# Quotient by remainder kept in PSUM, three banks for the first up-projection, v transposed mid-step, tokens stationary in the last product

## The chip, the cores and the metric

The kernel runs on one core of a Trainium2 chip. The metric is the device time of a run in microseconds. The engines are PE (TensorE, with PEld its weight loads), DVE (VectorE), ACT (ScalarE), POOL (GpSimd) and SP, which only issues transfers here.

## The reference

Channel attention over 6016 tokens of 256 channels, then two feed-forward layers of width 2048:

```python
qn = q / (norm(q, axis=tokens) + 1e-6);  kn = k / (norm(k, axis=tokens) + 1e-6)
x = v @ softmax(kn.T @ qn / tau)              # softmax with + 1e-9 in its divisor
h = x @ w_in1
P = a0 + a1*h + a2*h**2 + a3*h**3
Q = 1.0 + abs(b0)*abs(h) + abs(b1)*h**2
y = (P / (Q + 1e-6)) @ w_out1
h = y @ w_in2
out = (h * clip(h + 3, 0, 6) / 6) @ w_out2
```

All is float32. The attention matrix is folded into the first weight, so that v goes straight into the first up-projection.

## The kernel before

Products that must be exact to float32 are made of three matmuls: each operand is split into a rounded high part and the rest as a low part (`_hi`, `_lo`), and hi*hi, hi*lo and lo*hi are summed in PSUM (`split_product`, lines 334 to 336).

The first 66 us compute q'k, the softmax and the first columns of the folded weight. Then come steps t = 0, 1, ... over 13 blocks of tokens: one of 256, ten of 512, one of 384, one of 256. A step has 16 slots j, one for each chunk of 128 of the 2048 hidden features. The hidden features lie on the partitions, the tokens along the free axis. Each engine runs its own list, written out by hand, and counting semaphores tie the lists; a loop on the engine repeats the steps 3 to 9, the others are unrolled.

First stage, block t, chunk j: PE makes h in one of the two banks of H1 (`up1`, six matmuls). ACT reads it three times: T = a3*h + a2 (L563), SQ = |b1|*h*h (L565), AB = |b0|*|h| (L567). DVE makes T*h (`horner_2`, L750), (T + a1)*h (`horner_1`, L756) and SQ + AB (`q_body`, L764; on POOL, L295, in step 1). ACT takes the reciprocal square root of Q and squares it, which gives an approximate 1/Q in Y (L574, L580). DVE makes S = (T + a0)*Y (L771), E = Q*Y (L777) and G = (2 - E)*S (L784), one Newton step. ACT rounds G to g1_hi (L586), DVE subtracts to g1_lo (L792; on POOL, L301, for blocks 0 and 1). PE adds g1 times a part of w_out1 into YP (`down1`, six matmuls). T, SQ and g1 have four buffers, Y, AB and G two. These run with lags of 1, 2, 3 and 5 slots behind chunk j (`LAG_ROOT`, `LAG_NEWTON`, `LAG_SPLIT1`, `LAG_DOWN1`).

When all 16 chunks of a block are in YP, it is split to yT_hi (ACT, L605) and yT_lo (DVE, L804). Second stage, six slots behind (`SHIFT2`): `up2` into one of two banks of H2, R = relu(h + 3) (ACT, L592), R = min(R, 6)*h (DVE `gate2`, L798), g2_hi (ACT, L598), g2_lo (POOL, L307), and `down2`, which adds weights times tokens into OP, features on the partitions, three slots later. At the end of a block ACT scales OP into oT (L614), PE transposes it back into OP (`transpose_out`, L458), ACT copies it to o_tok (L621) and SP stores it.

v of the next block is transposed by PE at the end of a step into H1 (`transpose_v`, L370) and split by ACT (L540) and DVE (L724); there the first stage of the next block starts afresh. PSUM has eight banks, two for each of H1, H2, YP and OP.

## Time and profile before

| | |
|---|---|
| median of 3 runs | 1241.63 us (1241.12 to 1242.3) |
| span of the profiled execution | 1240.4 us |
| PE busy | 1165.5 us, 94%, 5440 matmuls |
| PEld busy | 954.5 us, 77% |
| DVE busy | 1156.9 us, 93%, 1723 instructions |
| ACT busy | 961.1 us, 77%, 1782 instructions |
| POOL busy | 360.6 us, 29%, 276 instructions |
| chain that ended last | PE 41%, DVE 37%, issue 18%, ACT 3% |

Busy time is an average over all stages. A matmul's row lasts until its result is out, so rows of matmuls overlap: their rate is read from start to start. Rows of DVE and ACT overlap their successor too, by 0.07 to 0.1 us, where it does not wait for them. In the timeline a row can stand for several instructions (x2).

### The profile page before, as it was taken

The page shows a single profiled execution, that of the slowest core. Times are in us where ns is not written, and L with a number is a line of the kernel's source. Part 1 is how long each engine was busy: PE and PEld are TensorE (multiplying, and loading weights), DVE is VectorE, ACT ScalarE, POOL GpSimd, SP SyncE. Part 2 cuts the span into 40 slices and gives each one's busy share as a digit, 9 for nine tenths or more (in the row PEclk, how much of TensorE's full clock was granted, in tenths as well). Part 3 has the DMA queues.
Part 4 walks back from the last instruction along what each step waited for, and adds up shares of the span by engine and source line. Part 5 has one row for each costly group of instructions (what it writes and reads, how often), then busy time and mean ns, then how long its engine had stood idle before and what let it go on. Part 6 is the DMA issues. An engine that isn't in the chain of part 4 may idle for free.

```text
span 1240.4 us, 17387 instructions
## 1 busy us (share of the span) xinstructions
PE 1165.5 (94%) x5440; PEld 954.5 (77%) x5440; DVE 1156.9 (93%) x1723; ACT 961.1 (77%) x1782; POOL 360.6 (29%) x276
## 2 busy tenths in 40 slices
PE   7876788899999999999999999999999999999998
PEld 6755566787787787787787787787787787888898
DVE  5779999999999999999999999999999999999872
ACT  6566787888887887887887887887887887787864
POOL 2146576222222222222222222222222222222334
PEclk9887899999999999999999999999999999999999
DMA  9730000000000000000000000000000000000000
GB/s 319 265 111 1 18 1 1 1 26 1 1 34 1 0 34 0 0 34 0 0 34 0 0 34 0 0 34 0 0 34 1 1 31 1 1 26 1 18 1 22
DMA packets 16210, 33.65 MB, mean 27 GB/s; under 512 B 1824, under 2 KB 6176, under 8 KB 15904
## 3 DMA queue, kind: packets, MB, share of 16 engines
q1 hardware_dynamic: 16160, 33.04, 7.5%
q8 instruction: 24, 0.39, 0.1%
q14 instruction: 26, 0.21, 0.1%
HBM read 26.87 MB, written 6.16 MB: 27 GB/s over the span
## 4 chain that ended last, share of the span: by engine, by line
PE 41%; DVE 37%; issue 18%; ACT 3%; DMA 0%; DVEq 0%; SPq 0%; POOL 0%; ACTq 0%
DVE T L771 7%; PE H L334 6%; DVE G L784 6%; DVE T L750 6%; PE H L336 6%; PE H L335 6%; DVE SQ L764 5%; DVE R L798 5%; DVE g_lo L792 4%; PE OP L343 3%; PE OP L334 3%; PE OP L336 3%; PE OP L335 3%; PE YP L334 3%; PE YP L336 3%
## 5 line engine op out<-in xcount | busy, mean ns | idle before, releaser
L307 POOL TENSOR_TENSOR g_lo<-R,g_hi 128x512 fp32r<-128x512 f32 (+2 forms) x208 | 267.1, 1285 | 754.9 <-ACT g_hi L598 754.9
L563 ACT ACTIVATE T<-H,coef 128x512 f32<-128x512 f32 (+2 forms) x208 | 153.0, 735 | 161.0 <-PE H L336 160.9
L777 DVE SCALAR_TENSOR_TENSOR Y<-SQ,Y 128x512 f32<-128x512 f32 (+2 forms) x208 | 206.0, 991 | 0.5
L334 PE MATMUL H<-vT_hi,wf_hi 128*128 128x512 f32 (+2 forms) x416 | 159.8, 384 | 20.6 <-DVE T L756 15.2
L334 PE MATMUL H<-yT_hi,wu_hi 128*128 128x512 f32 (+2 forms) x416 | 157.7, 379 | 11.2 <-DVE R L798 10.5
L764 DVE TENSOR_TENSOR SQ<-SQ,AB 128x512 f32<-128x512 f32 (+2 forms) x192 | 167.4, 872 | 0.0
L334 PE MATMUL YP<-g_hi,wd_hi 128*128 128x512 f32 (+2 forms) x416 | 160.0, 385 | 6.3 <-DVE yT_lo L804 5.6
L771 DVE SCALAR_TENSOR_TENSOR T<-T,coef,Y 128x512 f32<-128x512 f32 (+2 forms) x208 | 163.0, 784 | 0.0
L334 PE MATMUL OP<-g_hi,wd_hi 128*128 128x512 f32 (+2 forms) x416 | 156.8, 377 | 1.8 <-ACT o_tok L621 1.5
L336 PE MATMUL YP<-g_hi,wd_lo 128*128 128x512 f32 (+2 forms) x416 | 157.0, 377 | 0.0
L335 PE MATMUL YP<-g_lo,wd_hi 128*128 128x512 f32 (+2 forms) x416 | 156.9, 377 | 0.0
L335 PE MATMUL H<-vT_lo,wf_hi 128*128 128x512 f32 (+2 forms) x416 | 156.3, 376 | 0.0
L336 PE MATMUL H<-vT_hi,wf_lo 128*128 128x512 f32 (+2 forms) x416 | 156.0, 375 | 0.0
L336 PE MATMUL H<-yT_hi,wu_lo 128*128 128x512 f32 (+2 forms) x416 | 155.4, 373 | 0.0
L336 PE MATMUL OP<-g_hi,wd_lo 128*128 128x512 f32 (+2 forms) x416 | 155.4, 373 | 0.0
L335 PE MATMUL H<-yT_lo,wu_hi 128*128 128x512 f32 (+2 forms) x416 | 155.3, 373 | 0.0
L335 PE MATMUL OP<-g_lo,wd_hi 128*128 128x512 f32 (+2 forms) x416 | 155.2, 373 | 0.0
L798 DVE SCALAR_TENSOR_TENSOR R<-R,H 128x512 f32<-128x512 f32 (+2 forms) x208 | 130.0, 625 | 21.9 <-ACT R L592 21.7
L750 DVE TENSOR_TENSOR T<-T,H 128x512 f32<-128x512 f32 (+2 forms) x208 | 130.0, 625 | 18.6 <-ACT AB L567 18.5
L756 DVE SCALAR_TENSOR_TENSOR T<-T,coef,H 128x512 f32<-128x512 f32 (+2 forms) x208 | 142.5, 685 | 0.5
L784 DVE SCALAR_TENSOR_TENSOR G<-Y,T 128x512 f32<-128x512 f32 (+2 forms) x208 | 142.9, 687 | 0.0
L574 ACT ACTIVATE Y<-SQ 128x512 f32<-128x512 f32 (+2 forms) x208 | 125.4, 603 | 19.1 <-DVE G L784 18.5
(89 smaller groups left out, 2259.6 us busy)
## 6 DMA issues: line engine op xcount, KB each, us to landing
qk<-in_q SPq DMA_DIRECT2D x23, 256.0 KB, 5.6
qk<-in_k SPq DMA_DIRECT2D x23, 256.0 KB, 7.0
v_raw<-in_v SPq DMA_DIRECT2D x10, 512.0 KB, 3.6
out<-o_tok SPq DMA_DIRECT2D x10, 512.0 KB, 3.7
w_raw_b<-in_moe_w_out SPq DMA_DIRECT2D x8, 512.0 KB, 5.7
w_raw_a<-in_moe_w_in SPq DMA_DIRECT2D x1, 2048.0 KB, 11.5
w_raw_b<-in_moe_w_in SPq DMA_DIRECT2D x4, 512.0 KB, 6.1
v_raw<-in_v SPq DMA_DIRECT2D x2, 256.0 KB, 7.1
```

The costliest lines, as they stand in the source:

```text
L307: nc.gpsimd.tensor_tensor(g2_lo[:, j % 4, 0:w], R[:, j % 4, 0:w], g2_hi[:, j % 4, 0:w].bitcast(fp32), ALU.subtract).then_inc(g2_lo_done, 1)
L334: nc.tensor.matmul(psum, w_hi, x_hi, start=first, stop=False)
L335: nc.tensor.matmul(psum, w_hi, x_lo, start=False, stop=False)
L336: return nc.tensor.matmul(psum, w_lo, x_hi, start=False, stop=last)
L563: nc.scalar.activation(T[:, j % 4, 0:w], H1[:, j % 2, 0:w], ACT.Identity, bias=A2, scale=A3)
L750: nc.vector.tensor_tensor(T[:, j % 4, 0:w], T[:, j % 4, 0:w], H1[:, j % 2, 0:w], ALU.mult)\
L756: nc.vector.scalar_tensor_tensor(T[:, j % 4, 0:w], T[:, j % 4, 0:w], A1, H1[:, j % 2, 0:w], ALU.add, ALU.mult).then_inc(t3_done, 1)
L764: nc.vector.tensor_tensor(SQ[:, j % 4, 0:w], SQ[:, j % 4, 0:w], AB[:, j % 2, 0:w], ALU.add)\
L771: nc.vector.scalar_tensor_tensor(T[:, j % 4, 0:w], T[:, j % 4, 0:w], A0, Y[:, j % 2, 0:w], ALU.add, ALU.mult).then_inc(s_done, 1)
L777: nc.vector.scalar_tensor_tensor(Y[:, j % 2, 0:w], SQ[:, j % 4, 0:w], Q_CONST, Y[:, j % 2, 0:w], ALU.add, ALU.mult).then_inc(e_done, 1)
L784: nc.vector.scalar_tensor_tensor(G[:, j % 2, 0:w], Y[:, j % 2, 0:w], 2.0, T[:, j % 4, 0:w], ALU.subtract, ALU.mult, reverse0=True).then_in ...
L798: nc.vector.scalar_tensor_tensor(R[:, j % 4, 0:w], R[:, j % 4, 0:w], 6.0, H2[:, j % 2, 0:w], ALU.min, ALU.mult).then_inc(g2_done, 1)
```

## The change

- Quotient: the high part is g1_hi = (T3 + a0)*Y, rounded on being written. Then product = Q*g1_hi, rest = (T3 + a0) - product, and g1_lo = rest*Y. There is no Newton step on Y, no G, and ACT no longer rounds G. T3 (the result of `horner_1`) and the rest are written into the H1 bank of the chunk, which so stays in use until g1_lo is done.
- SQ + AB is always on POOL, `g1_split` is always on DVE (as `quotient_lo`), and POOL waits for the product of the slot before it splits g2.
- T and SQ have two buffers instead of four, g1 keeps four. `a1` of chunk j waits for g1_lo of chunk j-2.
- H1 has three banks, used in turn by the 16 chunks and the two halves of v, which are transposed after chunks 4 and 10; H2 has one bank; vT has two buffer pairs. The step takes a parity, and the loop holds two steps.
- `down2` has the tokens as the stationary operand and 256 columns of w_out2 as the moving one, so OP has the tokens on the partitions: `transpose_out` and `oT` are gone, `out_copy` scales.
- Lags: divide 1, down1 2, second stage 3, down2 2 behind it. The fold goes to OP instead of H2.

```diff
-    LAG_ROOT = 1
-    LAG_NEWTON = 2
-    LAG_SPLIT1 = 3
-    LAG_DOWN1 = 5
+    LAG_DIVIDE = 1
+    LAG_DOWN1 = 2
     SHIFT2 = LAG_DOWN1 + 1
-    LAG_DOWN2 = 3
+    LAG_DOWN2 = 2
+    V_BEHIND = 4, 10
+    RING = 3
...
-        T = sb("T", [P, 4, W], fp32)
-        G = sb("G", [P, 2, W], fp32)
-        SQ = sb("SQ", [P, 4, W], fp32)
+        T = sb("T", [P, 2, W], fp32)
+        SQ = sb("SQ", [P, 2, W], fp32)
...
-        H1, H2, YP, OP = ps("H1"), ps("H2"), ps("YP"), ps("OP")
+        H1, H2, YP, OP = ps("H1", RING), ps("H2", 1), ps("YP", 2), ps("OP", 2)
...
+        def place(j):
+            return j + sum(j > a for a in V_BEHIND)
+        def v_place(c):
+            return V_BEHIND[c] + 1 + c
+        def bank(at):
+            return at % RING
+        def wait_bank(engine, t, at):
+            before = at - RING
+            t, before = t + before // TURN, before % TURN
+            if not exists(t):
+                return
+            for c in range(CT):
+                if v_place(c) == before:
+                    if exists(t + 1):
+                        engine.wait_ge(vT_lo_done, CT * (t + 1) + c + 1)
+                    return
+            j = before - sum(before > v_place(c) for c in range(CT))
+            wait_chunk(engine, g1_lo_done, (t, j))
...
# POOL
+                    if exists(t):
+                        q_body(t, j)
...
+                    if x := stage(t - 1, j - SHIFT2):
+                        if y := stage(t, j - LAG_DIVIDE):
+                            wait_chunk(pool, product_done, y)
                         g2_split(*x)
...
# PE
-                if j >= 2:
-                    wait_chunk(pe, t3_done, (t, j - 2))
+                wait_bank(pe, t, place(j))
...
-                for d in range(CT):
-                    done = split_product(OP[:, d, 0:w], wd2_hi[:, j, d * P:(d + 1) * P],
...
+                for i in range(w // P):
+                    at = slice(i * P, (i + 1) * P)
+                    psum = OP[:, i // 2, i % 2 * C:(i % 2 + 1) * C]
+                    first, last = j == 0 and i % 2 == 0, j == J - 1
+                    nc.tensor.matmul(psum, g2_hi[:, j % 4, at], wd2_hi[:, j, :], start=first, stop=False,
+                                     skip_group_check=True)
...
# ACT
                 wait_chunk(act, u1_done, (t, j))
-                wait_chunk(act, g1_done, back(t, j, 4))
...
+                wait_chunk(act, g1_lo_done, back(t, j, 2))
+                nc.scalar.activation(T[:, j % 2, 0:w], h, ACT.Identity, bias=A2, scale=A3)
+                nc.scalar.activation(SQ[:, j % 2, 0:w], h, ACT.Square, scale=root_b1)
+                nc.scalar.activation(AB[:, j % 2, 0:w], h, ACT.Abs, scale=absb[:, 0:1]).then_inc(a1_done, 1)
...
# ACT, one slot
+                    if j == LAG_DOWN1 and exists(t - 1):
+                        yT_split(t - 1)
                     if u2:
                         c1(*u2)
+                    if exists(t):
+                        a1(t, j)
+                        if j in V_BEHIND and exists(t + 1):
+                            vT_split(t + 1, V_BEHIND.index(j), 1 - par)
+                    if x := stage(t, j - LAG_DIVIDE):
                         root(*x)
                         root_squared(*x)
+                    if u2:
+                        c2(*u2)
...
# DVE
+                nc.vector.scalar_tensor_tensor(h, T[:, j % 2, 0:w], A1, h, ALU.add, ALU.mult).then_inc(t3_done, 1)
...
+                nc.vector.scalar_tensor_tensor(g1_hi[:, j % 4, 0:w], H1[:, bank(place(j)), 0:w], A0, Y[:, j % 2, 0:w],
+                                               ALU.add, ALU.mult).then_inc(g1_hi_done, 1)
...
+                nc.vector.scalar_tensor_tensor(SQ[:, j % 2, 0:w], SQ[:, j % 2, 0:w], Q_CONST,
+                                               g1_hi[:, j % 4, 0:w].bitcast(fp32),
+                                               ALU.add, ALU.mult).then_inc(product_done, 1)
...
+                nc.vector.scalar_tensor_tensor(p, p, A0, SQ[:, j % 2, 0:w], ALU.add, ALU.subtract)\
+                  .then_inc(rest_done, 1)
...
+                nc.vector.tensor_tensor(g1_lo[:, j % 4, 0:w], H1[:, bank(place(j)), 0:w], Y[:, j % 2, 0:w], ALU.mult)\
+                  .then_inc(g1_lo_done, 1)
...
# DVE, one slot
+                    if j == LAG_DOWN1 and exists(t - 1):
                         yT_split(t - 1)
+                    if x := stage(t - 1, j - SHIFT2):
+                        gate2(*x)
+                    if exists(t):
+                        horner_2(t, j)
+                        horner_1(t, j)
+                        if j in V_BEHIND and exists(t + 1):
+                            vT_split(t + 1, V_BEHIND.index(j), 1 - par)
+                    if x := stage(t, j - LAG_DIVIDE):
+                        quotient_hi(*x)
+                        product(*x)
+                        rest(*x)
+                        quotient_lo(*x)
```

## Rows read from the trace of the kernel before

**Rows 1.** Busy time by stretch: from:to, length, busy us of each engine, clock.
```profile
104.00:114.00 10.00, 5.01 (x21) 4.72 (x22) 10.00 (x17) 3.96 (x12) 7.40 (x5) 0.59 0.00 0
170.00:180.00 10.00, 8.43 (x48) 6.74 (x47) 10.00 (x13) 7.86 (x16) 7.56 (x6) 1.00 0.01 2
500.00:600.00 100.00, 98.50 (x431) 78.72 (x430) 98.92 (x141) 80.57 (x142) 23.40 (x18) 1.00 0.03 10
```

**Rows 2.** Timeline of ACT, line 605: start us, duration, engine, what, idle before.
```profile
510.59 1.03 ACT L605 ACTIVATE yT_hi<-YP 128x1024 fp32r<-128x1024 f32 x1 [1.26 <-PE H L336]
...
603.90 1.03 ACT L605 ACTIVATE yT_hi<-YP 128x1024 fp32r<-128x1024 f32 x1 [1.26 <-PE H L336]
...
1148.40 0.81 ACT L605 ACTIVATE yT_hi<-YP 128x768 fp32r<-128x768 f32 x1 [1.82 <-PE H L336]
...
1205.93 0.60 ACT L605 ACTIVATE yT_hi<-YP 128x512 fp32r<-128x512 f32 x1 [2.39 <-PE H L336]
```

**Rows 3.** Timeline of PE: six matmuls in a full step, three behind a wait.
```profile
171.74 0.39 PE L334 MATMUL H<-yT_hi,wu_hi 128*128 128x256 f32 x1 [0.79 <-DVE R L798]
171.97 0.28 PE L335 MATMUL H<-yT_lo,wu_hi 128*128 128x256 f32 x1
172.08 0.28 PE L336 MATMUL H<-yT_hi,wu_lo 128*128 128x256 f32 x1
...
600.21 0.39 PE L334 MATMUL OP<-g_hi,wd_hi 128*128 128x512 f32 x1
...
601.61 0.39 PE L334 MATMUL YP<-g_hi,wd_hi 128*128 128x512 f32 x1
```

**Rows 4.** Timeline of ACT at the start of the 512-token block of step 1.
```profile
131.03 0.78 ACT L563 ACTIVATE T<-H,coef 128x512 f32<-128x512 f32 x1 [1.74 <-PE H L336]
...
132.28 0.68 ACT L567 ACTIVATE AB<-H,absb 128x512 f32<-128x512 f32 x1
```

**Rows 5.** Timeline of DVE at the same place.
```profile
132.99 0.69 DVE L750 TENSOR_TENSOR T<-T,H 128x512 f32<-128x512 f32 x1 [2.73 <-ACT AB L567]
133.72 0.75 DVE L756 SCALAR_TENSOR_TENSOR T<-T,coef,H 128x512 f32<-128x512 f32 x1
134.38 0.90 DVE L771 SCALAR_TENSOR_TENSOR T<-T,coef,Y 128x256 f32<-128x256 f32 x1
```

**Rows 6.** Groups by line and shape: busy us, mean ns, idle before.
```profile
L777 DVE SCALAR_TENSOR_TENSOR Y<-SQ,Y 128x512 f32<-128x512 f32 x160 | 167.9, 1049 | 0.3
L798 DVE SCALAR_TENSOR_TENSOR R<-R,H 128x512 f32<-128x512 f32 x160 | 108.0, 675 | 0.0
L574 ACT ACTIVATE Y<-SQ 128x512 f32<-128x512 f32 x160 | 103.2, 645 | 5.1 <-DVE G L784 5.0
L792 DVE TENSOR_TENSOR g_lo<-G,g_hi 128x512 fp32r<-128x512 f32 x144 | 98.6, 685 | 0.0
L295 POOL TENSOR_TENSOR SQ<-SQ,AB 128x512 f32<-128x512 f32 x16 | 24.1, 1508 | 13.8 <-ACT AB L567 13.7
```

**Rows 7.** Timelines of POOL and DVE in step 0, beside a weight split.
```profile
113.36 2.54 POOL L287 TENSOR_TENSOR wd_lo<-w_raw_b,wd_hi 128x1024 fp32r<-128x1024 f32 x1 [1.30 <-DVE wd_hi L743]
...
113.93 2.25 DVE L777 SCALAR_TENSOR_TENSOR Y<-SQ,Y 128x256 f32<-128x256 f32 x1
```

**Rows 8.** Timelines: ACT's first T, and DVE's last first-stage instruction.
```profile
66.32 0.56 ACT L563 ACTIVATE T<-H,coef 128x256 f32<-128x256 f32 x1 [2.25 <-PE H L336]
...
1199.29 0.88 DVE L792 TENSOR_TENSOR g_lo<-G,g_hi 128x256 fp32r<-128x256 f32 x1
```

**Rows 9.** Timelines of ACT and DVE in the last step, 256 tokens.
```profile
1188.58 0.57 ACT L563 ACTIVATE T<-H,coef 128x256 f32<-128x256 f32 x1 [0.49 <-PE H L336]
...
1189.40 0.47 ACT L567 ACTIVATE AB<-H,absb 128x256 f32<-128x256 f32 x1
...
1190.31 0.41 DVE L750 TENSOR_TENSOR T<-T,H 128x256 f32<-128x256 f32 x1
...
1190.97 0.47 DVE L756 SCALAR_TENSOR_TENSOR T<-T,coef,H 128x256 f32<-128x256 f32 x1
```

More of the change, by code:

```diff
@@ L201, in every_step, with h2 @@
             for t in steps[0]:
-                body(t)
-            with engine.Fori(*LOOP) as t:
-                body(t)
+                body(t, t % 2)
+            with engine.Fori(*LOOP, 2) as t:
+                body(t, LOOP[0] % 2)
+                body(t + 1, 1 - LOOP[0] % 2)
             for t in steps[1]:
-                body(t)
+                body(t, t % 2)
+        def place(j):
+            return j + sum(j > a for a in V_BEHIND)
+        def v_place(c):
+            return V_BEHIND[c] + 1 + c
+        TURN = J + CT
+        assert TURN % RING == 0
+        def bank(at):
[12 more added lines that the diff above has]
+            wait_chunk(engine, g1_lo_done, (t, j))
+        def h2(blk, j):
+            last = isinstance(blk, int) and blk == NB - 1
+            return (H1 if last and j % 2 else H2)[:, 0, 0:width(blk)]
         def stage(t, at):
@@ L257, in _, with step @@
                     load_weight(k, part)
-            def step(t):
-                if exists(t + 1) and not (isinstance(t, int) and t == 0):
-                    load_v(t + 1)
+            def step(t, par):
                 if exists(t - 2):
@@ L408, in up1 @@
                 for c in range(CT):
-                    done = split_product(H1[:, j % 2, 0:w], wf_hi[:, c, cols], wf_lo[:, c, cols],
-                                         vT_hi[:, c, 0:w], vT_lo[:, c, 0:w], c == 0, c == CT - 1)
+                    done = split_product(H1[:, bank(place(j)), 0:w], wf_hi[:, c, cols], wf_lo[:, c, cols],
+                                         vT_hi[par][:, c, 0:w], vT_lo[par][:, c, 0:w], c == 0, c == CT - 1)
                 done.then_inc(u1_done, 1)
@@ L428, in up2 @@
                 w = width(blk)
-                if at := back(blk, j, 2):
+                if at := back(blk, j, 2 if isinstance(blk, int) and blk == NB - 1 and j else 1):
                     wait_chunk(pe, g2_done, at)
@@ L532, in _, with vT_split @@
                                      accum_out=small[:, 26 + c:27 + c]).then_inc(exp_ready, 1)
-            def vT_split(blk):
+            def vT_split(blk, c, par):
                 w = width(blk)
-                for c in range(CT):
-                    act.wait_ge(vT_psum, CT * blk + c + 1)
-                    if not (isinstance(blk, int) and blk == 0) and c == 0:
-                        wait_chunk(act, u1_done, (blk - 1, J - 1))
-                    nc.scalar.activation(vT_hi[:, c, 0:w], H1[:, c, 0:w], ACT.Copy).then_inc(vT_hi_done, 1)
-            vT_split(0)
+                act.wait_ge(vT_psum, CT * blk + c + 1)
+                b = 1 + c if isinstance(blk, int) and blk == 0 else bank(v_place(c))
+                if c == 0 and exists(blk - 2):
+                    wait_chunk(act, u1_done, (blk - 2, J - 1))
+                nc.scalar.activation(vT_hi[par][:, c, 0:w], H1[:, b, 0:w], ACT.Copy).then_inc(vT_hi_done, 1)
+            for c in range(CT):
+                vT_split(0, c, 0)
             act.wait_ge(roots_taken, 1)
@@ L550, in fold_split @@
                     act.wait_ge(fold_made, CT * n + c + 1)
-                    nc.scalar.activation(wf_hi[:, c, columns(n)], H2[:, c, 0:PIECES[n] * P], ACT.Identity,
+                    nc.scalar.activation(wf_hi[:, c, columns(n)], OP[:, c, 0:PIECES[n] * P], ACT.Identity,
                                          scale=inverse_sum[:, c:c + 1])\
@@ L572, in root @@
                 wait_chunk(act, w_done, (blk, j))
-                wait_chunk(act, g1_done, back(blk, j, 2))
-                nc.scalar.activation(Y[:, j % 2, 0:w], SQ[:, j % 4, 0:w], ACT.Abs_reciprocal_sqrt, bias=Q_CONST)\
+                nc.scalar.activation(Y[:, j % 2, 0:w], SQ[:, j % 2, 0:w], ACT.Abs_reciprocal_sqrt, bias=Q_CONST)\
                    .then_inc(y_done, 1)
@@ new lines, in rest, with quotient_lo @@
+            def rest(blk, j):
+                w = width(blk)
+                p = H1[:, bank(place(j)), 0:w]
+                wait_chunk(dve, product_done, (blk, j))
+                nc.vector.scalar_tensor_tensor(p, p, A0, SQ[:, j % 2, 0:w], ALU.add, ALU.subtract)\
+                  .then_inc(rest_done, 1)
+            def quotient_lo(blk, j):
+                w = width(blk)
+                wait_chunk(dve, rest_done, (blk, j))
+                nc.vector.tensor_tensor(g1_lo[:, j % 4, 0:w], H1[:, bank(place(j)), 0:w], Y[:, j % 2, 0:w], ALU.mult)\
+                  .then_inc(g1_lo_done, 1)
```

250 lines of the change are left out of this document (64 added, 186 removed).

## The prediction

> **What bounds the kernel now.** I read three views in this order. First the busy time by stretches: in the body of the kernel PE is busy 98.5 of 100 us and DVE 98.9 of 100, ACT 81, POOL 23, at the full granted clock [rows 1]. Two engines are at their end together, so neither alone can be blamed from shares. Second, the timeline of ScalarE's copy of the finished YP, one per step: two of them are 93.3 us apart, which is the length of a step of 16 chunks of 512 tokens; the last two mark the 256-token block and the tail [rows 2]. Third, the timeline of PE: six 512-column matmuls take 1.40 us, 0.233 us each, and 256-column ones follow each other every 0.11 to 0.12 us, although each has its own weight load [rows 3]. A chunk has 24 matmuls of 512 columns, 5.6 us, and 16 chunks 89.5 us: PE's own work is 96% of the step. The rest is 16 transposes and short waits. DVE runs eight instructions a chunk of 0.68 to 0.75 us that overlap by 0.07 to 0.09 [rows 5, 6], about 5 us, and is filled up to 5.6 us because instructions with both inputs in SBUF stand behind POOL's (below). No engine waits for a round trip: ScalarE works on chunk j while VectorE divides chunk j-2 with four buffers between them.
>
> **The change, part by part.** *Work taken away.* DVE goes from eight instructions a chunk to seven (the sum SQ+AB goes to POOL, Newton's three and the split become quotient, product, remainder, low quotient). ACT goes from eight to seven (L586 is gone). PE loses eight output transposes a step with the waits around them. By work alone PE would be left with 89.5 us and eight transposes of v, some 0.8 us: 90.3 us a step. The product with tokens stationary has 12 matmuls of 256 columns for 6 of 512: 12 x 0.117 = 1.40 us, the same as 6 x 0.233, as long as weight loads stay hidden as in the 256-column rows [rows 3]. If they did not, 12 loads of 0.175 us (954.5 us by 5440) would make it 2.1 us, and PE 6.3 us a chunk.
>
> *The wait that is added.* T and SQ shrink from four buffers to two, and Y, SQ and g1 of a chunk now live until its last instruction. So L563's successor, the first ScalarE instruction of chunk j, waits for the low quotient of chunk j-2. On VectorE the order within slot j is: gate of the second stage, Horner twice for chunk j, then the four division instructions of chunk j-1. The low quotient of j-2 is therefore the last instruction of slot j-1, and nothing of slot j but the gate can run before ScalarE's three instructions on chunk j are through. Behind that wait on ScalarE stand root and its square of chunk j-1 and the copy g2_hi. That is a closed loop, ScalarE three instructions, VectorE six, ScalarE again, and its length is the slot:
> - ScalarE: from the start of T to the end of AB 1.93 us (131.03 to 132.96) [rows 4].
> - 0.03 us to VectorE (132.96 to 132.99). First Horner 0.69 and 0.04 to the second, which waits for it, start to start 0.73; the second to a next instruction that doesn't wait for it 0.66 [rows 5].
> - High quotient 0.74, product 0.69, remainder 0.74, low quotient 0.68, each waiting for the one before: 2.85 and three gaps of 0.04, 2.97. The values are those of instructions with the same inputs: 0.75 for one with a pointer scalar and PSUM, 0.68 otherwise [rows 5, 6]. The root and its square, 0.65 each behind AB, end about 1.2 us after AB, before the second Horner instruction lets go, so they add nothing.
> - 0.03 us back to ScalarE.
> Sum 1.93 + 0.03 + 0.73 + 0.66 + 2.97 + 0.03 = 6.35 us; I take 6.34. It is more than PE's 5.6 us.
>
> *Unknown: VectorE writing PSUM.* Second Horner and remainder now write to PSUM; no row of before shows that. The nearest rows are reads of PSUM, which cost nothing against SBUF: 675 ns with PSUM (L798), 685 without (L792) [rows 6]. I take 0. Below: the 0.07 us by which a VectorE row outlives its successor's start could go. Above: PE's rows, which end in PSUM, outlive it by 0.39 - 0.23 = 0.16 us [rows 3], 0.09 more. Two instructions a chunk, about 190 full chunks: -27 to +34 us.
>
> The Trainium skill, page "VectorE: DVE Perf Modes", section on the TRN2 errata, gives an instruction with a PSUM source 62 cycles more than one with SBUF sources, at 0.96 GHz. By the page five of the six VectorE instructions of the loop would be 0.065 us longer, an estimate of 0.32 us a chunk and a time of about 1510 us. The rows of L798 and L792 speak against it.
>
> *Three banks, and v in the ring.* The ring has 18 places a step, 16 chunks and two v transposes, at places 5 and 12. The up-projection at place p waits for the low quotient of place p-3. Without v between them that is chunk j-3, done a slot earlier. But chunks 5, 6, 11 and 12 have a v place within those three, so they wait for chunk j-2: the same event for which ScalarE waits. PE starts only then, and ScalarE gets its input after the six matmuls. Price at 512 columns: 0.05 us to PE, 0.1 us more for the first one's weight load [rows 3] (behind the wait 0.23 us to the second matmul instead of 0.12), 1.40 us for six, 0.16 us tail, 0.04 us to ScalarE, less the 0.03 that is already in the loop: 1.73 us, four times a step, 6.9 us. At 256 columns 1.15 us. Each v half also puts one VectorE instruction between Horner and quotient: 0.60 us, twice a step.
>
> *POOL.* The sum SQ+AB runs 1.5 us on POOL (L295) [rows 6]; it starts 1.96 us into the slot and ends at 3.5, before the product, the only VectorE instruction left with both inputs in SBUF, at about 4.1. The other POOL instruction waits for the product. So the long stretches that L777 shows (1049 ns in the mean, where L792, which also reads twice from SBUF, has 685) go away, but they were not on a loop of this kind. In step 0 POOL also splits weights, 2.5 us each, and one of before's 256-token instructions with both inputs in SBUF is 2.25 us long beside it [rows 7] where 0.41 is usual; there the product stands in the loop, +1.84 us in 8 slots, 14.7 us.
>
> *Hidden.* The YP copy and split (1.0 and 1.2 us) fit: ScalarE has 2 us to spare before its wait, VectorE has 1.9 us while ScalarE does the three. The v load is issued some ten slots ahead of its use, behind the output store on SP. With the cover gone they would cost up to 1.2 us a step.
>
> **The sum.** It is made against the profiled span of 1240.4 us; the median of the runs is 1.2 us above that.
> - Up to the first T: 66.3 us, as before [rows 8].
> - Step 0 (256 tokens). Loop at 256: T to end of AB 1.29 (1188.58 to 1189.87), VectorE instructions 0.41 or 0.47 long with 0.07 overlap [rows 9]: 1.29+0.03+0.46+0.39+0.51+0.45+0.51+0.41+0.03 = 4.08. 16 x 4.08 = 65.3, ring 4 x 1.15 = 4.6, v 1.2, POOL 14.7, fold splits and a half-speed PE about 5: 91 us. It was 131.0 - 66.3 = 64.7.
> - Steps 1 to 10: 16 x 6.34 + 1.2 + 6.9 = 109.5 each, 1095 us. It was 93.3.
> - The 384-token step, halfway between the two widths: 16 x 5.21 + 6.5 = 89.9. The last, 256: 65.3 + 4.6 = 69.9.
> - Last quotient 1.9. Tail 34, an estimate from 256-token durations: 3.7 for the last down-projection and the split of YP, 24 for 16 slots of PE at 1.40 (12 x 0.117) with a wait for an output copy, 2.3 for ScalarE, VectorE, ScalarE and POOL on the last chunk, 4 for its product, copy and store. It was 40, from 1200.2 to 1240.4 [rows 8], with longer lags and transposes.
> 66.3 + 91 + 1095 + 89.9 + 69.9 + 1.9 + 34 = 1448 us, as a run 1449 us.
>
> **The rivals.**
> - *The ring costs nothing* (the loop holds, the up-projections are early after all): 10 x 6.9 + 4.6 + 5.8 + 4.6 = 84 us less, 1365 us. For it: PE has idle time to work ahead. Against it: the bank's wait names the same low quotient. Chance 0.09.
> - *PE's clock falls* in the slots with the ring's wait, where PE is busy 5.6 of 8.1 us. At 1.2 GHz its 24 matmuls take 11.2 us and PE sets four slots a step, +12 us, 1570 us in all; dropping in half of them 1510. For it: the granted clock of 0.59 where PE was half busy (104 to 114 us). Against it: 1.00 at 8.4 of 10 us busy [rows 1]. Chance 0.10.
> - *The product with tokens stationary doesn't hide its loads*: PE 6.3 us a chunk, level with the loop, and with its own waits some 0.2 above it, 0.2 x 160 = 32, 1480 us; it lies within the range of the forecast. With it the forecast has 0.77.
> - *Faster: the loop does not bind.* If the six VectorE instructions together with ScalarE's three took under 5.6 us, PE would set the step again: 90.3 us for 93.3, ten times, and 6 us at the end: 1205 us. The point is 5.6 us a slot; the rows give 6.34, and it would take 0.12 us less for each of the six. Chance 0.04.
>
> **How the numbers follow.** The forecast's own range is 1410 to 1495 us (the PSUM writes, the loads, step 0). To leave no more than 2 in 10 outside, the range goes down to the first rival: 1360 to 1495. Slower by over 0.2% holds the forecast and the first three rivals, 0.95; faster 0.04; within 0.2%, about what can be told from no change here, 0.01.
>
> **What the profile of the changed kernel would show.** The loop: T starting 0.03 us behind the low quotient of j-2, the first Horner instruction idle until AB, slots of 6.3 us. The ring: a matmul of H behind a wait for the low quotient, and slots of 8 us, at chunks 5, 6, 11 and 12. DVE's busy share near 75%, PE's near 80%, the clock at 1.00. YP copies 109 to 110 us apart. 256-column matmuls into OP every 0.117 us. I am wrong if T starts behind a matmul throughout, if the steps are near 90 us, or if DVE has no gaps.

## The result, and the profile after

| | before | after |
|---|---|---|
| median of 4 runs each (lowest to highest), us | 1241.38 (1239.71 to 1242.3) | 1483.22 (1481.53 to 1484.3) |
| after / before, 95% interval | | 1.1946 (1.1929 to 1.1963) |
| span of the profiled execution, us | 1240.4 | 1479.4 |
| length of a full step, us | 93.3 | 112.7 (mean of ten, 111.0 to 114.4) |

The forecast was 1449 us in a range of 1360 to 1495. The time lies inside, on the side it was forecast to, 34 us above the number. A version with the same instructions in another order, found on the way, takes 1196.93 us and is faster than both kernels (the experiment gate_first).

The page of the kernel after: busy time and instructions of each engine, then the chain of work that ended last.

```profile
span 1479.4 us, 18228 instructions
...
PE 1232.5 (83%) x6354; PEld 1037.3 (70%) x6354; DVE 1022.5 (69%) x1563; ACT 880.3 (60%) x1561; POOL 522.7 (35%) x436
...
DVE 46%; ACT 24%; PE 18%; issue 10%; DMA 0%; ACTq 0%; SPq 0%; POOL 0%; DVEq 0%; POOLq 0%
```

No engine is full any more, yet the chain names DVE and ACT in turn. That is the sign of a closed loop: work passes from one to the other and each waits in between. The busy time of the same 100 us as in [rows 1] shows it too. Columns as there.

```profile
500.00:600.00 100.00, 85.47 (x424) 70.45 (x422) 70.67 (x103) 61.50 (x104) 36.66 (x29) 0.95 0.03 11
```

One turn of the loop, in the timelines of DVE and ACT in step 5 (start, duration, engine, line, what, idle before):

```profile
703.24 0.78 ACT L574 ACTIVATE T<-H,coef 128x512 f32<-128x512 f32 x1 [2.31 <-DVE g_lo L775]
703.92 0.68 ACT L575 ACTIVATE SQ<-H,root_b 128x512 f32<-128x512 f32 x1
704.49 0.69 ACT L576 ACTIVATE AB<-H,absb 128x512 f32<-128x512 f32 x1
...
709.68 0.78 ACT L574 ACTIVATE T<-H,coef 128x512 f32<-128x512 f32 x1 [2.31 <-DVE g_lo L775]
```

```profile
705.21 0.69 DVE L737 TENSOR_TENSOR T<-T,H 128x512 f32<-128x512 f32 x1 [1.47 <-ACT AB L576]
705.93 0.76 DVE L744 SCALAR_TENSOR_TENSOR H<-T,coef,H 128x512 f32<-128x512 f32 x1
706.60 0.74 DVE L752 SCALAR_TENSOR_TENSOR g_hi<-H,coef,Y 128x512 fp32r<-128x512 f32 x1
707.37 0.69 DVE L759 SCALAR_TENSOR_TENSOR SQ<-SQ,g_hi 128x512 f32<-128x512 f32 x1
708.10 0.76 DVE L768 SCALAR_TENSOR_TENSOR H<-H,coef,SQ 128x512 f32<-128x512 f32 x1
708.89 0.69 DVE L775 TENSOR_TENSOR g_lo<-H,Y 128x512 fp32r<-128x512 f32 x1
```

AB ends at 705.18 and Horner's first starts at 705.21; the low quotient of j-2 ends at 709.58 and T of the next chunk starts at 709.68. From T to T it is 6.44 us. It is the place of the rows in [rows 4] and [rows 5]. Both engines now idle in each slot: DVE 1.5 us for AB, ACT 2.3 us for the low quotient.

At chunks 5, 6, 11 and 12 the first ScalarE instruction waits for PE instead, and PE for the same low quotient. Timelines of ACT and PE at chunk 5 of step 6:

```profile
751.63 0.78 ACT L574 ACTIVATE T<-H,coef 128x512 f32<-128x512 f32 x1 [3.18 <-PE H L360]
```

```profile
749.92 0.50 PE L358 MATMUL H<-vT_hi,wf_hi 128*128 128x512 f32 x1 [2.16 <-DVE g_lo L775]
```

Summed over the run, the waits give the size of each link (who waits, for whom, us in total, times, longest):

```profile
DVE T L737 <- ACT AB L576: 376.5, 204, 4.7
...
ACT T L574 <- DVE g_lo L775: 275.8, 138, 4.0
ACT T L574 <- PE H L360: 187.2, 69, 5.8
...
PE H L358 <- DVE g_lo L775: 106.4, 50, 4.5
```

### The profile page after: what moved, and what is told of

It reads as the page before. It is cut to its first block, busy times and chain, and to the rows that moved or that the text cites. A ratio compares the mean times of both kernels' runs of the same rounds, so it can differ in the third digit from the quotient of the medians.

```text
span 1479.4 us, 18228 instructions
## 1 busy us (share of the span) xinstructions
PE 1232.5 (83%) x6354; PEld 1037.3 (70%) x6354; DVE 1022.5 (69%) x1563; ACT 880.3 (60%) x1561; POOL 522.7 (35%) x436
## 4 chain that ended last, share of the span: by engine, by line
DVE 46%; ACT 24%; PE 18%; issue 10%; DMA 0%; ACTq 0%; SPq 0%; POOL 0%; DVEq 0%; POOLq 0%
DVE H L768 9%; DVE SQ L759 9%; DVE g_hi L752 9%; ACT T L574 8%; DVE g_lo L775 8%; DVE T L737 8%; ACT SQ L575 7%; ACT AB L576 7%; PE H L358 4%; PE H L360 3%; PE H L359 3%; PE OP L367 3%; DVE vT_lo L707 1%; DVE H L744 1%; PE OP L480 1%
## 5 line engine op out<-in xcount | busy, mean ns | idle before, releaser
L325 POOL TENSOR_TENSOR SQ<-SQ,AB 128x512 f32<-128x512 f32 (+2 forms) x208 | 247.8, 1191 | 595.8 <-ACT AB L576 595.8
L737 DVE TENSOR_TENSOR T<-T,H 128x512 f32<-128x512 f32 (+2 forms) x208 | 132.3, 636 | 376.6 <-ACT AB L576 376.5
L480 PE MATMUL OP<-wd_hi,g_hi 128*128 128x256 f32 x752 | 221.9, 295 | 0.9 <-POOL g_lo L331 0.8
L482 PE MATMUL OP<-wd_lo,g_hi 128*128 128x256 f32 x752 | 219.5, 292 | 0.0
L484 PE MATMUL OP<-wd_hi,g_lo 128*128 128x256 f32 x752 | 217.3, 289 | 0.0
L358 PEld LDWEIGHTS H<-vT_hi,wf_hi 128*128 128x128 f32 x416 | 83.6, 201 | 148.5 <-DVE g_lo L775 126.7
L593 ACT ACTIVATE R<-H 128x512 f32<-128x512 f32 (+2 forms) x208 | 114.1, 549 | 86.1 <-PE H L360 84.5
L480 PEld LDWEIGHTS OP<-wd_hi,g_hi 128*128 128x128 f32 x752 | 150.2, 200 | 8.3 <-POOL g_lo L331 1.5
L482 PEld LDWEIGHTS OP<-wd_lo,g_hi 128*128 128x128 f32 x752 | 150.1, 200 | 6.6
L768 DVE SCALAR_TENSOR_TENSOR H<-H,coef,SQ 128x512 f32<-128x512 f32 (+2 forms) x208 | 147.2, 708 | 7.3
L744 DVE SCALAR_TENSOR_TENSOR H<-T,coef,H 128x512 f32<-128x512 f32 (+2 forms) x208 | 146.6, 705 | 7.4
```

Source lines behind the costliest of these rows:

```text
L325: nc.gpsimd.tensor_tensor(SQ[:, j % 2, 0:w], SQ[:, j % 2, 0:w], AB[:, j % 2, 0:w], ALU.add)\
L358: nc.tensor.matmul(psum, w_hi, x_hi, start=first, stop=False)
L480: nc.tensor.matmul(psum, g2_hi[:, j % 4, at], wd2_hi[:, j, :], start=first, stop=False, skip_group_check=True)
L482: nc.tensor.matmul(psum, g2_hi[:, j % 4, at], wd2_lo[:, j, :], start=False, stop=False, skip_group_check=True)
L484: done = nc.tensor.matmul(psum, g2_lo[:, j % 4, at], wd2_hi[:, j, :], start=False, stop=last, skip_group_check=True)
L737: nc.vector.tensor_tensor(T[:, j % 2, 0:w], T[:, j % 2, 0:w], H1[:, bank(place(j)), 0:w], ALU.mult)\
```

## The experiments

The theory going in: two things cost the time, the loop through ScalarE and VectorE (6.44 us a slot where PE needs 5.6), and the wait of the bank ring at four chunks a step. A third, smaller, is PE's clock. Rivals were that instructions became dearer (writing PSUM, 256-column matmuls), or that a single swap in the order is to blame. Kernels compared with one another ran beside runs of the kernel before whose medians are 1241.1 to 1243.7 us. order_act, order_dve, buffers3, ring4, banks4 and no_ab were run once each; kernels run four times or more spread by at most 0.6%, and the differences read below are larger than that, except that order_act's 4 us is no difference.

**tokens_only.** The last product with tokens stationary, put alone into the kernel before.

```diff
-                for d in range(CT):
-                    done = split_product(OP[:, d, 0:w], wd2_hi[:, j, d * P:(d + 1) * P],
-                                         wd2_lo[:, j, d * P:(d + 1) * P], g2_hi[:, j % 4, 0:w],
-                                         g2_lo[:, j % 4, 0:w], j == 0, j == J - 1)
+                for i in range(w // P):
+                    at = slice(i * P, (i + 1) * P)
+                    psum = OP[:, i // 2, i % 2 * C:(i % 2 + 1) * C]
...
-            def transpose_out(blk):
```

> The kernel before with one part of the change alone: tokens stationary in the last product, no transposes back, one copy of OP that scales. Theory: 12 matmuls of 256 columns cost what 6 of 512 do, and eight transposes and the waits for two copies go, 1.0 to 2.0 us a step: 91.3 to 92.3 us, 1222 to 1233 us. Rival (twice as many weight loads are not hidden): PE's slot grows by 0.7 us, 1350 us.

Measured 1229.79 us, ratio 0.9887 (0.9868 to 0.9907); a step is 92.6 us (copies of YP at 600.39 and 692.95), 0.8 us less than before where 1.0 to 2.0 were expected. So this part is not the loss: it gains 1.1%, 14 us. In the kernel after its matmuls still follow each other every 0.12 us, with loads hidden:

```profile
751.55 0.28 PE L482 MATMUL OP<-wd_lo,g_hi 128*128 128x256 f32 x1
751.67 0.28 PE L484 MATMUL OP<-wd_hi,g_lo 128*128 128x256 f32 x1
```

**order_act, order_dve, order_both.** Is it the order alone? ScalarE does root and square of chunk j-1 ahead of T of chunk j (order_act); VectorE does the division of j-1 ahead of the split of YP, the gate and Horner (order_dve); or both.

```diff
+                    if x := stage(t, j - LAG_DIVIDE):
+                        root(*x)
+                        root_squared(*x)
                     if exists(t):
                         a1(t, j)
```

```diff
+                    if x := stage(t, j - LAG_DIVIDE):
+                        quotient_hi(*x)
+                        product(*x)
+                        rest(*x)
+                        quotient_lo(*x)
                     if j == LAG_DOWN1 and exists(t - 1):
                         yT_split(t - 1)
```

> Only ACT's list is reordered (root and square of chunk j-1 before the three instructions on chunk j). Theory: the loop goes from ACT's three through Horner and the division as before, 6.44 us a slot; no change, 1475 to 1490 us. Rival (root and square stand in the way): 1.2 us a slot less, about 1290 us.

> Only DVE's list is reordered (division of chunk j-1 before gate and Horner of chunk j). Theory: the loop stays closed through ACT, where root and square of j-1 stand behind the three instructions on j: 0.1 + 1.8 + 1.3 + 3.0 = 6.2 us a slot against 6.44, and the ring's 1.7 us stays: steps of 108 to 110 us, about 1445 us. Rival (DVE's order alone is what counts): near 93 us a step and 1240 us.

> The changed kernel with two lists reordered and nothing else: in each slot DVE does the four division instructions of chunk j-1 before the gate and Horner of chunk j, and ACT does root and its square of chunk j-1 before the three instructions on chunk j. Theory (the loop of ACT's three and DVE's six instructions sets the slot): the wait for the low quotient of j-2 is then answered 4.9 us of DVE work before Horner needs its result, the loop spans two slots and costs about 3.9 us each, so PE's 5.6 us sets the slot and the ring's wait is covered too: steps of 90 to 93 us, 1210 to 1245 us in all. Rival (POOL's share of SBUF and the ring of banks are what costs): the product now runs beside POOL's instructions and the up-projections of chunks 5, 6, 11 and 12 still wait: steps above 100 us, over 1350 us.

Measured: order_act 1487.05, as expected. order_dve 2362.65 and order_both 1535.85 (ratio 1.2348, 1.2311 to 1.2384): both far off. The new order of both lists does take T out of the old loop, but I had not looked at the second stage. It has one bank, H2. Its matmuls wait for the gate that reads the bank. ScalarE's R, which needs those matmuls, stands ahead of the root. The division waits for the root, and the gate now stands behind the division. Timelines of DVE, PE, ACT and again DVE of order_both:

```profile
708.19 0.68 DVE L781 SCALAR_TENSOR_TENSOR R<-R,H 128x512 f32<-128x512 f32 x1
```

```profile
708.92 0.51 PE L358 MATMUL H<-yT_hi,wu_hi 128*128 128x512 f32 x1 [1.30 <-DVE R L781]
```

```profile
710.62 0.60 ACT L593 ACTIVATE R<-H 128x512 f32<-128x512 f32 x1 [1.09 <-PE H L360]
711.12 0.62 ACT L581 ACTIVATE Y<-SQ 128x512 f32<-128x512 f32 x1
```

```profile
712.44 0.75 DVE L752 SCALAR_TENSOR_TENSOR g_hi<-H,coef,Y 128x512 fp32r<-128x512 f32 x1 [2.19 <-ACT Y L587]
...
715.36 0.68 DVE L781 SCALAR_TENSOR_TENSOR R<-R,H 128x512 f32<-128x512 f32 x1
```

Gate to PE 0.73, to R 1.70, to the root 0.50, to its square 0.65, to the quotient 0.67, to the next gate 2.92: 7.17 us, the new slot (708.19 to 715.36). In order_dve root and square stand behind T, SQ and AB, and T waits for its up-projection, which PE has behind the second one's: the same round with another six matmuls and three activations in it, slots of 11.2 us and more. The clock is in this too: in one such slot the twelve matmuls start at 1139.76 us and T behind them at 1145.29, where twelve take 2.8 us at the rate of [rows 3]. That kernel's clock was 0.80 in the mean.

**gate_first.** The loop of order_both, and no other, is broken by putting the gate back ahead of the division. ScalarE as in order_act; VectorE: YP split, gate, division of j-1, Horner of j.

```diff
                         gate2(*x)
-                    if exists(t):
-                        horner_2(t, j)
-                        horner_1(t, j)
-                        if j in V_BEHIND and exists(t + 1):
-                            vT_split(t + 1, V_BEHIND.index(j), 1 - par)
                     if x := stage(t, j - LAG_DIVIDE):
                         quotient_hi(*x)
                         product(*x)
                         rest(*x)
                         quotient_lo(*x)
+                    if exists(t):
+                        horner_2(t, j)
+                        horner_1(t, j)
```

> As order_both, but DVE does the gate of the second stage ahead of the four division instructions. Theory: order_both opened the loop through T and closed another through the one bank of H2 (gate, up-projection of the second stage, ACT's R, root, square, division, gate: 0.7 + 1.7 + 0.5 + 0.7 + 0.7 + 2.9 = 7.2 us, which is its slot). With the gate first the division is out of that loop, what remains of it is 0.7 + 1.7 + 0.6 = 3.0 us, the loop through T spans two slots, and the bank that chunks 5, 6, 11 and 12 wait for comes free 3.6 us into the slot instead of at its end. PE's 5.6 us sets the slot: 91 to 94 us a step, 1215 to 1250 us. Rival (any order of these lists costs more than the old one, since product and POOL now overlap in SBUF): above 5.9 us a slot, over 1290 us.

Measured 1196.93 us, ratio 0.9625 (0.9603 to 0.9647), a little better than expected. With the same count of instructions as the kernel after (18228) it is 286 us faster. Steps are 90.6 to 91.9 us (copies of YP at 485.08, 575.76 and 667.41). Windows, and the timeline of ACT:

```profile
500.00:600.00 100.00, 100.00 (x536) 85.33 (x536) 89.21 (x128) 75.56 (x129) 45.87 (x36) 1.00 0.05 17
```

```profile
515.26 0.76 ACT L574 ACTIVATE T<-H,coef 128x512 f32<-128x512 f32 x1
...
519.18 0.60 ACT L593 ACTIVATE R<-H 128x512 f32<-128x512 f32 x1 [1.48 <-PE H L360]
...
520.87 0.76 ACT L574 ACTIVATE T<-H,coef 128x512 f32<-128x512 f32 x1
```

T no longer waits for the low quotient: the division of j-1 follows the gate at once, so that the low quotient of j-2 is over long before. PE is busy all the time, at 5.61 us a slot. The loss was the order, given two buffers and three banks. In this order the whole change is a gain of 47 us, of which the tokens stationary gave 14 alone; what the quotient and the v transposes amid the step each give was not separated.

**buffers3.** The same order as the kernel after, but three buffers of T and SQ. The wait for the low quotient of j-2 moves from T to the root, which writes Y.

```diff
-        T = sb("T", [P, 2, W], fp32)
-        SQ = sb("SQ", [P, 2, W], fp32)
+        T = sb("T", [P, 3, W], fp32)
+        SQ = sb("SQ", [P, 3, W], fp32)
...
-                wait_chunk(act, g1_lo_done, back(t, j, 2))
```

> The lists are as in the changed kernel; T and SQ get three buffers, used in turn with the banks of H1, and ACT's wait for the low quotient of j-2 goes from the three instructions to root. Theory: 12 slots of a step are no longer in the loop and take PE's 5.6 us, the four whose bank comes from chunk j-2 stay at 8.1: 12 x 5.6 + 4 x 8.1 + 1.2 = 101 us a step, about 1345 us. Rival (the loop isn't the wait but DVE's own seven instructions with what POOL holds them up): 112 us a step as now.

Measured 1369.57 us, 25 more than expected. Most slots outside the ring's chunks are 5.61 us; the ring's stay (8.70 and 8.10 us from T to T). The timeline of ACT at chunk 12 of step 6, with T of chunk 11 at 729.05 and T of chunk 13 at 742.76:

```profile
737.15 0.78 ACT L572 ACTIVATE T<-H,coef 128x512 f32<-128x512 f32 x1 [3.29 <-PE H L359]
```

So the loop goes with the third buffer, and the ring is a cause of its own. Without the loop a ring slot stands out by 2.5 us instead of 1.66, as the expectation had it (8.1 for 5.6). The 25 us lie elsewhere, in ten steps of 103.5 us in the mean instead of 101: about 10 us in the slots at chunk 2, where YP is split (6.4 us and more instead of 5.61), 4 us in two slots of 7.8 us where the loop on the engine goes back to its start (below), and most of the rest in ring slots and those behind them, at a granted clock of 0.59 to 0.98.

**ring4.** Four banks, with the two buffers of the kernel after. Room is made by adding the token tiles of the last product two by two into one bank, so that this kernel, and the two with four banks below, leave out the separation of these tiles in the output. 18 places a step are no multiple of four, so two empty places were put at the end of the turn.

```diff
-    RING = 3
+    RING = 4
...
-        TURN = J + CT
+        TURN = J + CT + 2
```

> The changed kernel with four banks for the first up-projection, so that no chunk waits for the bank of chunk j-2. The bank comes from OP: all four token tiles of the last product are added into one bank, so that part of the output is not computed as the reference has it, with the same instructions; the copy of OP is two instructions. Theory: the four ring waits of 1.66 us a step and most of the slow-clock slots behind them go, the loop of 6.44 us stays: 16 x 6.44 + 1.2 = 104.2 us a step for 112.7, about 1390 us. Rival (the ring costs nothing): 1480 us.

Measured 1437.08 us: a miss by 47. The waits at chunks 5, 6, 11 and 12 had gone, but two new ones had come. The empty places shortened the ring at the turn of the step, so that chunks 0 and 1 waited for chunks 14 and 15 of the step before, j-2 again. Timeline of ACT at chunks 0 and 1 of step 6:

```profile
694.17 0.78 ACT L580 ACTIVATE T<-H,coef 128x512 f32<-128x512 f32 x1 [5.32 <-PE H L366]
...
702.28 0.78 ACT L580 ACTIVATE T<-H,coef 128x512 f32<-128x512 f32 x1 [1.98 <-PE H L366]
```

It says where the wait goes when two places of the ring stay empty, but it doesn't price a ring without this wait. So once more:

**banks4 and banks4_buffers3.** No empty places: the bank goes by the running count of places, and the order of the banks alternates from step to step. Alone, and with the three buffers.

```diff
+            odd[0] = par
...
-            return at % RING
+            return (TURN * odd[0] + at) % RING
```

> The changed kernel with four banks for the first up-projection and no empty places: the bank is taken by the running count of places (18 a step), so the order of banks alternates between even and odd steps. To make room the last product adds its token tiles two by two into one bank, so two tiles of the output are mixed; number and size of the matmuls stay the same, the output copy becomes two of half the size. A place then waits for the low quotient four places back, which is chunk j-3 even with a v transpose in between. Theory (the wait of chunks 5, 6, 11 and 12 is the v place within three banks): all slots 6.44 us, steps of 16 x 6.44 + 1.2 = 104.2 us plus what the clock takes, 105 at most; 1482 - 10 x 8 - 14 for the two ragged steps and step 0: 1388 us, between 1380 and 1400. Rival (these slots wait for something else that a fourth bank doesn't free, as the transposes themselves): the 8.1 us slots stay and the time is 1470 or more.

> The same four banks (two tiles of the output mixed, as there) together with three buffers of T and SQ, taken by place. The wait for the low quotient of j-2 moves from T to the root, except at chunks 5, 6, 11 and 12, where the buffer of T was last used by chunk j-2, so that ScalarE waits there for it, though PE no longer does. Theory (the loop and the ring are the whole loss): 12 slots of 5.61 us, four of 6.44, 1.2 us of v: 94.3 us a step, about 18 us less a step than the changed kernel; 1482 - 180 - 25 at the ends: about 1265 us, between 1235 and 1285, and a granted clock of 0.98 or more. Rival (the two losses overlap, or a third wait comes next): over 1300 us.

Measured 1386.64 and 1264.79 us (the second with ratio 1.0182, 1.0154 to 1.0209), both in the expected range (the granted clock of the second, 0.974, lies below the 0.98 expected). The timeline of ACT in banks4 at chunks 5 and 6, where T waits for VectorE and no more for PE:

```profile
741.91 0.78 ACT L586 ACTIVATE T<-H,coef 128x512 f32<-128x512 f32 x1 [2.43 <-DVE g_lo L789]
...
748.36 0.78 ACT L586 ACTIVATE T<-H,coef 128x512 f32<-128x512 f32 x1 [2.32 <-DVE g_lo L789]
```

The four slots are 7.04, 6.44, 7.04 and 6.44 us, as long as the others but for the 0.60 of a v half. Steps are 104.0 to 105.1 us with one of 106.8, against 112.7. With three buffers besides, full steps are 93.9 to 95.2 us but for the first (87.1) and two of 98.5 and 99.9, which have a slot of 9.6 and one of 11.0 us at their end. Those are the places where the loop on the engine, which holds two steps, turns, that is, goes back to its start, behind steps 4 and 6: in the first, PE stands still for 2.07 us ahead of the second stage's matmuls at 507.06 and waits for nothing that the profile shows, and the granted clock is 0.82. The kernel after has the same pause there (below); what PE does in it stays open. Buffers alone take 114 us away, banks alone 97, and both 218: the two losses add up, they don't hide each other.

**no_ab.** The third ScalarE instruction, AB, left out, to price the loop by its links.

```diff
-                nc.scalar.activation(AB[:, j % 2, 0:w], h, ACT.Abs, scale=absb[:, 0:1]).then_inc(a1_done, 1)
```

> The changed kernel without ACT's third instruction on a chunk (AB = |b0|*|h|); POOL adds SQ to itself instead, so the divisor is not the reference's. ACT is busy 60% of the span. Theory: ACT's three instructions are in the loop at their full time, start to start 0.57 us for this one, so the slot goes from 6.44 to 5.87 us, a step from 112.7 to 103.5, and 190 chunks save about 105 us: near 1378 us. The ring's four waits stay. Rival (an engine that is 60% busy sets nothing): 1480 us.

Measured 1359.78 us. Slots are 5.86 us (T at 704.20 and 710.06), 0.58 less, and AB puts off the end of ScalarE's part by as much (704.60 to 705.18 above): an engine busy 60% of the span gives back all that an instruction adds to the loop. That was expected; the time is 18 us better than expected, and the clock, of which the expectation said nothing, is 0.970 in the mean instead of 0.941.

```profile
704.20 0.78 ACT L574 ACTIVATE T<-H,coef 128x512 f32<-128x512 f32 x1 [1.05 <-DVE g_lo L774]
```

**swap_waits.** T has two waits, for the up-projection and for the low quotient, and starts 0.10 us behind the latter, not 0.03. Does the order of the two waits matter?

```diff
-                wait_chunk(act, u1_done, (t, j))
-
                 wait_chunk(act, g1_lo_done, back(t, j, 2))
+                wait_chunk(act, u1_done, (t, j))
```

> The changed kernel with ACT's two waits in front of T in the other order, the low quotient of j-2 first, the up-projection second. In the changed kernel T starts 0.09 to 0.10 us behind the low quotient's end, where other instructions of ACT start 0.03 behind VectorE. Theory (the last of two waits, when it is the one that is late, costs 0.06 more): 0.06 us less in 12 slots of a step, about 8 us of 1483, ratio to before lower by 0.007. Rival (the gap is that of this pair of engines): no difference.

Measured 1477.82 us, ratio 1.1901 (1.1877 to 1.1924) against 1.1946 (1.1929 to 1.1963): 5 us less, of 8 expected. The trace says where. The timelines of DVE and ACT in step 9, which is unrolled:

```profile
1059.36 0.69 DVE L774 TENSOR_TENSOR g_lo<-H,Y 128x512 fp32r<-128x512 f32 x1
```

```profile
1060.09 0.78 ACT L573 ACTIVATE T<-H,coef 128x512 f32<-128x512 f32 x1 [2.25 <-DVE g_lo L774]
```

The low quotient ends at 1060.05 and T starts 0.04 us behind it. It is 0.03 to 0.05 us in all the unrolled steps (0 to 2 and 9 to 12), where the kernel after has 0.09 to 0.10, and the slots are 6.38 instead of 6.44. In the ring's slots, where the up-projection, now the second wait, is the late one, T starts 0.10 us behind PE instead of 0.04, and the slot grows from 8.10 to 8.16. So in these steps the theory holds: the second of two waits, when it is the late one, costs 0.06 us more, whichever engine it is for. In the steps inside the loop on the engine (3 to 8) the swap gains nothing: the gap to the low quotient is 0.11 to 0.13 us, and the slots are 6.46:

```profile
702.96 0.78 ACT L573 ACTIVATE T<-H,coef 128x512 f32<-128x512 f32 x1 [2.34 <-DVE g_lo L774]
```

Here the low quotient ends at 702.85 (702.16 + 0.69). Why the steps inside the loop differ stays open.

## Why the prediction was right, and where its sizes were off

**The mechanism was right.** The added wait closes a loop of ScalarE and VectorE. T waits for the low quotient, Horner for AB; one buffer more (buffers3) removes it, one instruction less (no_ab) shortens it by what that instruction adds. The price of instructions was as read from the rows: tokens stationary at 0.12 us for 256 columns [rows 3], high quotient 0.745, product 0.69 [rows 6]; only the sum on POOL took 1.30 us, not 1.5, and it is not in the loop. The ring's price of 1.73 us was 1.66.

**Where the 31 us of the span come from.** The sum against the trace, by the starts of T (208 of them; a step is 16):

| stretch | forecast | measured | from |
|---|---|---|---|
| up to the first T | 66.3 | 64.6 | T at 64.55 |
| step 0 | 91 | 87.8 | T at 152.35 |
| steps 1 to 10 | 1095 | 1127.2 | T at 1279.52 |
| the 384-token step | 89.9 | 91.7 | T at 1371.17 |
| last step, quotient, tail | 105.8 | 108.2 | end at 1479.4 |

The ten steps carry it all. Three terms:
- *The loop was 6.44, not 6.34:* 160 x 0.10 = 16 us. Of the 0.10, 0.06 to 0.07 is the way back from the low quotient to T, for which I took 0.03 from the way from AB to VectorE [rows 4, 5]. No row of before showed ScalarE's T released by VectorE. In the unrolled steps swap_waits shows the reason: the low quotient is the second of T's two waits. The rest, 0.03 us, is 0.01 here and there: the sum came to 6.35 and was taken as 6.34, and writing PSUM costs a little, below. At 256 tokens the loop was 4.20 us for 4.08, at 384 5.32 for 5.21.
- *The ring:* 40 x (1.66 - 1.73) = -3 us.
- *The clock,* which the sum took as 1.00. The ten steps are 160 x 6.44 + 40 x 1.66 + 12 (v) = 1108.8 us, and 18.4 us are left. They lie in a few intervals from T to T: 18 of 160 are 0.5 to 1.7 us above 6.44, 8.10 or 8.70, whichever is theirs, and hold 17.6 us. In all 18 the granted clock is 0.57 to 0.93. It is low, 0.74 to 0.98, in 20 other intervals too, and those are longer by 0.2 us at most: a low clock costs where the slot waits for the matmuls that it falls on. Eleven of the 18 are ring slots (9.4 us), five lie at chunk 2, where PE has waited 1.8 to 3.2 us for the split of YP (4.8 us), and two, of 8.17 and 8.15 us, at the turn of the loop on the engine behind steps 4 and 6 (3.4 us). In these two the clock is not alone: PE first stands still for 1.93 us, and what it waits for the profile doesn't show ("issue"):

```profile
600.54 0.49 PE L358 MATMUL H<-yT_hi,wu_hi 128*128 128x512 f32 x1 [1.93 <-issue]
```

The windows of the interval of 9.96 us at chunk 5 of step 1, and of the one ahead of it:

```profile
170.00:177.00 7.00, 3.86 (x19) 2.88 (x18) 5.12 (x9) 3.66 (x7) 2.03 (x2) 1.00 0.00 0
177.00:187.00 10.00, 6.69 (x24) 5.50 (x25) 5.43 (x9) 4.17 (x8) 2.01 (x2) 0.57 0.00 0
```

I had put the clock among the rivals as a thing of 12 us a step, or of half the ring slots; it is some 1.7 us a step.

A place where it falls, in the timeline of PE and the windows at chunk 6 of step 6:

```profile
758.37 0.39 PE L359 MATMUL H<-vT_lo,wf_hi 128*128 128x512 f32 x1
758.60 0.49 PE L360 MATMUL H<-vT_hi,wf_lo 128*128 128x512 f32 x1
758.88 0.63 PE L358 MATMUL H<-vT_hi,wf_hi 128*128 128x512 f32 x1
759.31 0.63 PE L359 MATMUL H<-vT_lo,wf_hi 128*128 128x512 f32 x1
```

```profile
756.00:758.00 2.00, 0.00 (x0) 0.00 (x0) 1.93 (x4) 0.44 (x1) 1.26 (x1) 1.00 0.00 0
758.00:760.00 2.00, 1.97 (x6) 1.59 (x7) 0.57 (x1) 0.00 (x0) 0.00 (x0) 0.69 0.00 0
760.00:762.00 2.00, 2.00 (x10) 1.90 (x10) 0.00 (x0) 1.60 (x3) 0.00 (x0) 0.50 0.00 0
```

The granted clock is 1.00 (2.4 GHz) while PE waits, and 0.50 (1.2 GHz) from 758.9 on: the matmuls go from one every 0.23 us to one every 0.43. PE had been idle for 2.2 us before the matmul at 758.03. It had been for as long a slot earlier, ahead of 749.92, and there the clock stayed at 1.00, so the idle time alone does not tell when it falls. The low clock falls into six matmuls on which a ring slot hangs; the slot is 8.77 us for 8.10. The low clock doesn't last. The row that spoke against the rival, 1.00 at 8.4 us busy in 10 [rows 1], was thus no safe ground, and the rival's price was too high because it let the clock fall in each ring slot and stay.

**VectorE writing PSUM.** Taken at 0 between -27 and +34 us. The groups by line and shape (busy us, mean ns of one, idle before):

```profile
L768 DVE SCALAR_TENSOR_TENSOR H<-H,coef,SQ 128x512 f32<-128x512 f32 x160 | 121.4, 759 | 5.6
L744 DVE SCALAR_TENSOR_TENSOR H<-T,coef,H 128x512 f32<-128x512 f32 x160 | 120.9, 756 | 5.7
L752 DVE SCALAR_TENSOR_TENSOR g_hi<-H,coef,Y 128x512 fp32r<-128x512 f32 x160 | 119.2, 745 | 0.0
L759 DVE SCALAR_TENSOR_TENSOR SQ<-SQ,g_hi 128x512 f32<-128x512 f32 x160 | 110.7, 692 | 5.5
L775 DVE TENSOR_TENSOR g_lo<-H,Y 128x512 fp32r<-128x512 f32 x160 | 110.6, 691 | 5.6
```

L744 and L768 write PSUM and take 756 and 759 ns; L752, with the same pointer scalar and an output in SBUF, takes 745. So it is 0.01 us each, 4 us in all: the value of 0 was nearly right, the bounds too wide. The same instruction in the kernel before, L756 with its output in SBUF, took 736, but L750, which the change left as it was (L737 after), went from 676 to 688 as well, so that this comparison too leaves 0.01 us. L775 reads PSUM and L759 doesn't, and they take the same, 691 and 692 ns. The term of 62 cycles that the Trainium skill, page "VectorE: DVE Perf Modes", section "The TRN2 errata", gives for a PSUM source does not show here: by it, an estimate, the time would have been about 1510 us. The Trainium skill's (N+151)/0.96 ns in the same section, given for an fp32 tensor_tensor add, comes to 691 ns for 512 elements. L775, a product of two tensors, takes just that, with one of its sources in PSUM.

**POOL.** In the body the product is never stretched: 692 ns in the mean of 160, where L777 had 1049 [rows 6]. In step 0 it is, beside POOL's weight splits; timelines of POOL and DVE:

```profile
70.45 2.34 POOL L319 TENSOR_TENSOR wu_lo<-w_raw_b,wu_hi 128x1024 fp32r<-128x1024 f32 x1
```

```profile
71.09 1.98 DVE L759 SCALAR_TENSOR_TENSOR SQ<-SQ,g_hi 128x256 f32<-128x256 f32 x1
...
92.01 0.42 DVE L759 SCALAR_TENSOR_TENSOR SQ<-SQ,g_hi 128x256 f32<-128x256 f32 x1
```

Six of the 16 products are 1.9 to 2.0 us long and one is 1.40, so 10.3 us against the 14.7 forecast. That is more than the 3.2 us by which step 0 came out shorter; the 256-token loop of 4.20 us instead of 4.08 took 1.9 of it back.

**The rivals.** The ring that costs nothing did not happen, and banks4 shows what it would have given, 1387 us (1365 forecast). The loads of the 256-column matmuls stay hidden. The loop that does not bind is what gate_first made: PE sets the step at 90.6 to 91.9 us, 1197 us (forecast for that case: 90.3 and 1205). Of the signs named ahead, T behind the low quotient, ring slots of 8.1 us at the four chunks, the idle time of the first Horner instruction and the 256-column matmuls every 0.12 us were there, with DVE at 69% of the span and PE at 83%. Off were the clock at 1.00, the gap of 0.03 us ahead of T (0.10) and with both the steps of 109 to 110 us (112.7).

My largest misses were behind the forecast, in the experiments: order_dve and order_both were expected faster and came out slower, because I broke one loop and did not walk the others. The single bank H2 closes one as soon as the gate stands behind anything that waits for the root.

## What to carry to other kernels

Where engines work through lists in a fixed order and hand buffers round, list each wait with what stands ahead of the waiting instruction and ahead of its releaser, walk every cycle through them, and add up its length per slot; the longest of these and the busiest engine's work set the slot. Fewer buffers or another order change which cycles exist, not what an instruction costs, so a change that takes work away from VectorE and ScalarE and adds none to PE cost 19% here, and the same instructions in another order gained 4%. Do this for each order again, for all the stages that share an engine: breaking one cycle readily closes another.
